# A three-stage attention and mixture kernel: weight mixing moved into the attention loop, query loads put ahead of value loads, keys stored once per tile

## The chip, the cores and the metric

The kernel runs on one core of a Trainium2 chip. The metric is the device time of one execution in microseconds (us); lower is better.

## What is computed

The reference is three stages, each feeding the next. Cut to what matters:

```python
# 1. chunked attention, B=2, H=8, S=768, D=64, with 8 memory keys
for c in range(S // 32):
    q_c = q[:, :, c*32:(c+1)*32]
    k_ctx = k[:, :, max(0, c*32-16):min(S, c*32+32+8)]     # v_ctx likewise
    k_full = np.concatenate([mem_k, k_ctx], axis=2)        # 64 keys
    scores = scale * np.matmul(q_c, k_full.transpose(0, 1, 3, 2))
    scores = scores - np.max(scores, axis=-1, keepdims=True)
    a = np.exp(scores); a = a / (np.sum(a, axis=-1, keepdims=True) + 1e-09)
    out[:, :, c*32:(c+1)*32] = np.matmul(a, v_full)
# 2. channel mixing, x is (2, 768, 512)
xk = mu_k * x + (1.0 - mu_k) * x_prev                      # xr likewise
k = np.maximum(xk @ w_k, 0.0)                              # 512 -> 1024
out = sigmoid(xr @ w_r) * (k * k @ w_v)                    # 512 -> 512, 1024 -> 512
# 3. top-1 of 8 experts per token, with a sequential rule for keeping the last expert
h = np.maximum(x[b, s] @ w1[e], 0.0); out[b, s] = p[e] * (h @ w2[e])
```

## The kernel before

The 1536 tokens are 12 tiles of 128 rows. Each engine has its own instruction stream, written out by hand, and the streams meet at semaphores; there is no scheduler. Pairs of tiles are one round of a loop: `over_pairs` runs round 0, then rounds 1 to 4 as a loop, then round 5. `u` (0 or 1) is the tile's place in its pair and picks the buffer.

**Attention, one tile t.** TensorE (PE) transposes the probabilities of tile t (`probs_transposed`, L343, four 128x128 transposes), computes the scores of tile t+2 (`scores`, L330), transposes the normalised output of tile t-1 (`x_transposed`, L368) and multiplies probabilities by values (`values`, L357). Scores and values are 32 small matmuls each, of 64 rows and 32 columns of the array; a fp32 matmul leaves two records in the trace. VectorE (DVE) takes maxima and subtracts them (`shifted`, L765 and L775), then normalises (`normed`, L784, L790, L795). ScalarE (ACT) copies the transposed probabilities out of PSUM (L576), copies the transposed output (L582) and takes the exponentials of tile t+2 (L570).

**Its loads.** SyncE (SP) issues all of them in order on one queue. `QK` holds a tile's queries (512 words a partition) and keys. The keys are laid out by the host as four windows of 64 keys for each head pair, 8 memory keys and 56 others in each, so neighbouring windows repeat keys: 1024 words. `VV` holds the values, 1040 words. Both have two buffers. `QK` of tile t+4 may be loaded when the scores of tile t+2 are done, and `VV` of tile t+2 when `values` of tile t is done; SP waits for the second first:

```python
def ahead(t, u, more=True):
    sp.wait_ge(pv_done, t + 1)
    v_load(t + 2, u)
    if more:
        sp.wait_ge(scores_done, t + 3)
        qk_load(t + 4, u)
```

`probs_transposed` of tile t waits for the exponentials of t, `VV` of t and, in all but the last pair, `QK` of t+2.

**Weights of the channel mixing.** They come as 10 chunks of 128x1024 (`RAW`, two buffers, from `wmix`). ACT rounds each into `WHI` (`weight_hi`, L588) and DVE subtracts to get `WLO` (`weight_lo`, L805); each product is then three matmuls, high by high, high by low and low by high. The ten loads are queued behind the last value load. Four chunks are converted in the last attention pair, two after each tile; the other six inside the first round of the mixing. The products there are `up` (L403), `gate` (L419), `down` (L435). The mixing's inputs are made by ACT (`mix_scaled`, L616; `mix_hi`, L627) and DVE (`mix_full`, L812; `mix_lo`, L820). For pair 0 this stands in the last attention pair, behind the first tile's two weight chunks, and ahead of the copy L576 that the last tile's `values` needs. `up` waits for four chunks of `WLO` and for the last copy L582. Later `x2_transposed` (L445) needs `X2F` from DVE (L876), and `logits` (L453) are four fp32 matmuls with a 128x128 stationary operand and nine moving columns.

**Constants.** `CO` (940 words a partition) holds the identity used by all transposes and the tables of the routing. Every engine waits for all of it, and for two small tensors that ACT loads, `MU` and `WG` (`const_in` at 48).

**Experts.** After the routing, each expert's weights are loaded, split and multiplied (L513, L530). The change leaves this stage alone.

Of the kernel before, what the change touches and what calls it, by code (L numbers as in the profile page):

```python
# [33 lines left out]
VW = DH + 1  # L34
QW, KW, VWT = HP * P, HP * CPT * KEYS, HP * CPT * VW
INW = QW + KW + VWT
NPAIR = NT // 2
# [22 lines left out]
def moe_program(nc, tiles, wmix, mus, wgate, wexp, consts, out):  # L60
    ctx = ExitStack()
    with ctx:
# [58 lines left out]

        QK = [place(f"QK{i}", [P, QW + KW]) for i in range(2)]
        VV = [place(f"VV{i}", [P, VWT]) for i in range(2)]
# [32 lines left out]

        const_in = sem("const_in")
        qk_loaded = [sem(f"qk_loaded{i}") for i in range(2)]
        v_loaded = [sem(f"v_loaded{i}") for i in range(2)]
# [83 lines left out]
        @block.sync  # L243
        def _(sp):
            def qk_load(t, u):
                sp.dma_start(QK[u][:], tiles[ds(t, 1), :, 0:QW + KW].rearrange("a p n -> (a p) n")
                             ).then_inc(qk_loaded[u], 16)

            def v_load(t, u):
                sp.dma_start(VV[u][:], tiles[ds(t, 1), :, QW + KW:INW].rearrange("a p n -> (a p) n")  # L250
                             ).then_inc(v_loaded[u], 16)

            def raw_load(n, u):
                sp.dma_start(RAW[u][:], wmix[:, ds(n * CH1, CH1)]).then_inc(raw_loaded[u], 16)

            qk_load(0, 0)
            sp.dma_start(CO[:], consts).then_inc(const_in, 16)
            qk_load(1, 1)
            v_load(0, 0)
            v_load(1, 1)  # L260

            def ahead(t, u, more=True):

                sp.wait_ge(pv_done, t + 1)
                v_load(t + 2, u)
                if more:
                    sp.wait_ge(scores_done, t + 3)
                    qk_load(t + 4, u)

            for t in range(2):  # L270
                sp.wait_ge(scores_done, t + 1)
                qk_load(t + 2, t)
            with sp.Fori(0, NPAIR - 2) as g:
                ahead(2 * g, 0)
                ahead(2 * g + 1, 1)
# [38 lines left out]
        def _(pe):  # L314
# [3 lines left out]
            def scores(t, u, first):  # L318
# [5 lines left out]
                q = QK[u][:, 0:QW].rearrange("p (h n) -> p h n", h=HP)  # L324
                k = QK[u][:, QW:QW + KW].rearrange("p (h c n) -> p h c n", h=HP, c=CPT)
# [61 lines left out]

            pe.wait_ge(wlo_done, N1A)
            pe.wait_ge(xt_evac, NT)
# [18 lines left out]
            def gate(g, u, first):  # L408
                pe.wait_ge(xlo_done[1], g + 1)
                if first:  # L410
                    pe.wait_ge(wlo_done, N1A + KT * D // CH1)
                else:
                    pe.wait_ge(sig_done, 2 * g + u - 1)
# [10 lines left out]
            def down(g, u, first):  # L424
# [4 lines left out]
                for f in range(FT):  # L429
                    c = WV0 + f * D  # L430
                    if first and c % CH1 == 0:
                        pe.wait_ge(wlo_done, c // CH1 + 1)
                    r = slice(u * P, u * P + P)
# [46 lines left out]


            pe.wait_ge(route_step, R_FLAGS)
            nc.tensor.transpose(PS[0][0:NT, 0:P], RN[3][:], ident)
# [81 lines left out]
        def _(act):  # L565
# [19 lines left out]

            def weight_hi(n):
                act.wait_ge(raw_loaded[n % 2], 16 * (n // 2 + 1))
                nc.scalar.activation(WHI[:, n * CH1:(n + 1) * CH1], RAW[n % 2][:],  # L588
                                     ACT.Copy).then_inc(whi_done, 1)

            def attention(g, first, last):
                for u in range(2):
# [69 lines left out]
            def mix(g, first, last):  # L662
# [97 lines left out]
        def _(dve):  # L760
# [40 lines left out]

            def weight_lo(n):
                dve.wait_ge(whi_done, n + 1)
                c = slice(n * CH1, (n + 1) * CH1)
                nc.vector.tensor_tensor(WLO[:, c], RAW[n % 2][:], WHI[:, c].bitcast(F32),  # L805
                                        ALU.subtract).then_inc(wlo_done, 1)
# [16 lines left out]
            def attention(g, first, last):  # L823
                for u in range(2):
# [14 lines left out]
            nc.vector.tensor_scalar(OM[:], MU[:], -1.0, 1.0, ALU.mult, ALU.add)  # L839
            nc.vector.tensor_copy(X2R[:, :, D + 1], CO[:, C_TOK:C_TOK + NT])  # L840
            nc.vector.memset(ZR[:, 0:D + 1], 0.0)
# [36 lines left out]
            def mix(g, first, last):  # L878
                squared(g, 0, first)
                if not first:  # L880
                    logits_out(2 * g - 2)
                if first:
                    weight_lo(N1A)
                squared(g, 1, first)
                if not first:
                    logits_out(2 * g - 1)
                else:
                    weight_lo(N1A + 1)
                squared(g, 2, first)
                if first:  # L890
                    weight_lo(N1A + 2)
                squared(g, 3, first)
                if first:
                    for n in range(N1A + 3, N1):
                        weight_lo(n)
                if not last:
# [241 lines left out]
def _layout(q, k, v, mem_k, mem_v):  # L1138
# [5 lines left out]
    qt = q.reshape(B, HP, 2, ntb, P, DH).transpose(0, 3, 2, 5, 1, 4).reshape(NT, P, QW)  # L1144
    kw = np.empty((B, H, nch, KEYS, DH), k.dtype)
    vw = np.zeros((B, H, nch, KEYS, VW), v.dtype)
    kw[:, :, :, :] = mem_k[:, :, None, 0:1]
    for c in range(nch):
        lo, hi = max(0, c * CHUNK - LEFT), min(S, (c + 1) * CHUNK + RIGHT)
        at = NMEM + lo - (c * CHUNK - LEFT)  # L1150
        kw[:, :, c, 0:NMEM] = mem_k
        kw[:, :, c, at:at + hi - lo] = k[:, :, lo:hi]
# [4 lines left out]
    kt = kw.reshape(B, HP, 2, ntb, CPT, KEYS, DH).transpose(0, 3, 2, 6, 1, 4, 5).reshape(NT, P, KW)  # L1157
    vt = vw.reshape(B, HP, 2, ntb, CPT, KEYS, VW).transpose(0, 3, 2, 5, 1, 4, 6).reshape(NT, P, VWT)
    return np.ascontiguousarray(np.concatenate([qt, kt, vt], axis=2))

# [49 lines left out]
```

## Time and profile before

| what | value |
|---|---|
| median of 3 runs | 531.41 us (528.64 to 531.82) |
| profiled execution | 533.26 us, its span 531.5 us |
| busy in the span | PE 440.0, DVE 245.9, ACT 212.7, POOL 55.3 us |
| mean granted TensorE clock | 0.919 of 2.4 GHz |
| moved by DMA | 67.31 MB |

The span runs from the first to the last instruction of the profiled execution; its own time is 1.8 us longer. Times within the trace count from the span's start. A granted clock of 1.00 is 2.4 GHz and 0.50 is 1.2 GHz. The chain of waits follows the last instruction back to what released it; an entry there is work or a transfer that nothing hid. A DMA's entry in it starts at its issue and ends when it has landed.

### The profile page before, as it was taken

Reading aid. Unit: us, or ns where it says so; the run is one execution under the profiler, and the core shown is the slowest. Engines: PE = TensorE matmul, PEld = TensorE weight load, DVE = VectorE, ACT = ScalarE, POOL = GpSimd, SP = SyncE. Lnnn points to the kernel's source line nnn. Section 1 sums busy time; section 2 is a strip of 40 time slices with the busy share of each in tenths; the row PEclk is TensorE's granted clock in tenths of the full one; section 3 lists DMA queues with packets and bytes.
Section 4 is the critical chain, followed back from the end, with each engine's and each line's share of the span. In section 5 each row is a group of like instructions: output and inputs, shape, how many; then the busy total and the mean of one; then the engine's idle time right before and its main releaser. Section 6 shows DMA issues by size and latency. Waiting matters only on the chain.

```text
span 531.5 us, 10141 instructions
## 1 busy us (share of the span) xinstructions
PE 440.0 (83%) x3759; PEld 366.4 (69%) x3759; DVE 245.9 (46%) x477; ACT 212.7 (40%) x319; POOL 55.3 (10%) x62
## 2 busy tenths in 40 slices
PE   1667628999999999999940069999999999999993
PEld 1545518889898989989830047777777777777772
DVE  2454575653535234354045149222382247464861
ACT  1333474663435253344022038222462245555750
POOL 0000000010100101010003601111111111111110
PEclk9967867999999999999975569999999999999998
DMA  8668442428000000000004779511173128383810
GB/s 302 253 208 294 157 181 86 152 90 309 0 0 0 0 0 0 0 0 1 2 0 158 238 281 406 209 54 40 52 227 136 40 71 253 141 251 132 271 61 10
DMA packets 18313, 67.31 MB, mean 127 GB/s; under 512 B 2734, under 2 KB 2734, under 8 KB 18288
## 3 DMA queue, kind: packets, MB, share of 16 engines
q1 hardware_dynamic: 13104, 50.92, 27.9%
q0 software_dynamic: 4896, 16.05, 8.8%
q8 instruction: 15, 0.25, 0.2%
q14 instruction: 10, 0.08, 0.0%
q10 hardware_dynamic: 288, 0.02, 0.0%
HBM read 55.41 MB, written 12.62 MB: 128 GB/s over the span
## 4 chain that ended last, share of the span: by engine, by line
PE 67%; DMA 14%; issue 7%; DVE 5%; POOL 3%; ACT 2%; SPq 1%; POOLq 0%; DVEq 0%; ACTq 0%
PE PS L530 16%; PE PS L403 12%; PE PS L513 12%; PE PS L435 10%; DMA QK<-tiles 5%; PE PS L419 5%; DMA XR<-grouped_rows 5%; POOL grouped_rows L1107 2%; PE PS L521 2%; PE PS L453 2%; PE PS L504 1%; PE PS L330 1%; PE PS L357 1%; DMA RAW<-wmix 1%; PE PS L343 1%
## 5 line engine op out<-in xcount | busy, mean ns | idle before, releaser
L1022 DVE TENSOR_TENSOR ELO<-ERAW,EHI 128x1024 fp32r<-128x1024 f32 x56 | 66.8, 1219 | 12.9 <-ACT EHI L696 10.3
L696 ACT ACTIVATE EHI<-ERAW 128x1024 fp32r<-128x1024 f32 x56 | 57.4, 1053 | 29.6 <-DMA ERAW<-wexp 20.8
L403 PE MATMUL PS<-XHI,WHI 128*128 128x256 f32 x192 | 56.6, 295 | 1.2 <-DVE WLO L805 1.2
L530 PE MATMUL PS<-EHI,HH 128*128 128x512 f32 x128 | 54.6, 426 | 2.6 <-issue 1.0
L403 PE MATMUL PS<-XHI,WLO 128*128 128x256 f32 x192 | 55.2, 287 | 0.0
L403 PE MATMUL PS<-XLO,WHI 128*128 128x256 f32 x192 | 55.1, 287 | 0.0
L513 PE MATMUL PS<-EHI,XSH 128*128 128x512 f32 x128 | 53.0, 414 | 1.4 <-DVE XSL L1030 1.4
L1043 DVE TENSOR_TENSOR HL<-PS,HH 128x512 fp32r<-128x512 f32 x32 | 22.1, 691 | 66.3 <-ACT HH L716 65.9
L513 PE MATMUL PS<-ELO,XSH 128*128 128x512 f32 x128 | 51.5, 402 | 0.0
L513 PE MATMUL PS<-EHI,XSL 128*128 128x512 f32 x128 | 51.2, 400 | 0.0
L530 PE MATMUL PS<-EHI,HL 128*128 128x512 f32 x128 | 50.6, 395 | 0.0
L530 PE MATMUL PS<-ELO,HH 128*128 128x512 f32 x128 | 50.5, 395 | 0.0
L857 DVE TENSOR_TENSOR KK<-KR 128x512 f32<-128x512 f32 x24 | 16.6, 692 | 53.3 <-ACT KR L643 53.2
L1123 POOL DMA_INDIRECT rows_out<-OSB,OIDX x16 | 20.4, 1274 | 185.0 <-DVE OIDX L1077 185.0
L711 ACT ACTIVATE HS<-PS 128x512 f32<-128x512 f32 x32 | 19.1, 596 | 50.0 <-PE PS L513 50.0
L403 PEld LDWEIGHTS PS<-XHI,WHI 128*128 128x128 f32 x192 | 37.7, 196 | 1.6 <-issue 1.6
L403 PEld LDWEIGHTS PS<-XHI,WLO 128*128 128x128 f32 x192 | 37.8, 197 | 0.0
L403 PEld LDWEIGHTS PS<-XLO,WHI 128*128 128x128 f32 x192 | 37.7, 196 | 0.0
L435 PE MATMUL PS<-WHI,KHI 128*128 128x512 f32 x96 | 37.5, 390 | 0.1
L435 PE MATMUL PS<-WHI,KLO 128*128 128x512 f32 x96 | 37.4, 389 | 0.0
L435 PE MATMUL PS<-WLO,KHI 128*128 128x512 f32 x96 | 37.3, 389 | 0.0
L504 PE MATMUL PS<-CO,XR 128*128 128x128 f32 x68 | 10.9, 284 | 31.1 <-DMA XR<-grouped_rows 31.1
(141 smaller groups left out, 774.6 us busy)
## 6 DMA issues: line engine op xcount, KB each, us to landing
ERAW<-wexp SPq DMA_DIRECT2D x56, 512.0 KB, 5.6
QK<-tiles SPq DMA_DIRECT2D x12, 768.0 KB, 5.7
VV<-tiles SPq DMA_DIRECT2D x12, 520.0 KB, 3.9
grouped_rows<-ZR POOLq DMA_DIRECT2D x1, 5140.0 KB, 18.1
RAW<-wmix SPq DMA_DIRECT2D x10, 512.0 KB, 3.8
XR<-grouped_rows POOLq DMA_DIRECT2D x17, 257.0 KB, 4.2
CO<-consts SPq DMA_DIRECT2D x1, 470.0 KB, 6.5
rows_out<-OSB,OIDX POOLq DMA_INDIRECT x16, 3.9
```

The source lines that it names most:

```text
L403: last = nc.tensor.matmul(PS[q % 2][:, half * 256:half * 256 + 256], w[:, c:c + P], x[:, k, :], start=n == 0, stop=n == 11)
L419: last = nc.tensor.matmul(PS[2 + u][:, :], x[:, k, r], w[:, c:c + D], start=n == 0, stop=n == 11)
L435: last = nc.tensor.matmul(PS[4 + u][:, :], x[:, f, r], w[:, c:c + D], start=n == 0, stop=n == 23)
L504: last = nc.tensor.transpose(PS[5][:, k * P:(k + 1) * P], XR[:, k * P:(k + 1) * P], ident)
L513: last = nc.tensor.matmul(PS[part][:, :], x[:, k, :], ww[:, c:c + 512], start=n == 0, stop=n == 11)
L530: last = nc.tensor.matmul(PS[4][:, :], x[:, f, :], ww[:, c:c + D], start=n == 0, stop=n == 23)
L696: nc.scalar.activation(EHI[w][:, c * CH2:(c + 1) * CH2], ERAW[c][:], ACT.Copy).then_inc(ehi_done, 1)
L711: nc.scalar.activation(HS[:, part * 512:part * 512 + 512], PS[part][:, :], ACT.Relu).then_inc(hrelu_done, 1)
L857: nc.vector.tensor_tensor(KK[q % 2][:], KR[q % 2][:], KR[q % 2][:], ALU.mult).then_inc(kk_done, 1)
L1022: nc.vector.tensor_tensor(ELO[w][:, c * CH2:(c + 1) * CH2], ERAW[c][:], EHI[w][:, c * CH2:(c + 1) * CH2].bitcast(F32), ALU.subtract).then_ ...
L1043: nc.vector.tensor_tensor(HL[:, 4 * part:4 * part + 4, :].rearrange("p k n -> p (k n)"), PS[2 + part][:, :], HH[:, 4 * part:4 * part + 4, ...
L1123: pool.indirect_dma_start(out, bass.IndirectOffsetOnAxis(ap=OIDX[:, 0:1], axis=0), OSB[:], None, bounds_check=last_row, oob_is_err=False). ...
```

## The change

All 10 chunks are converted in the attention: one `weight_hi` and one `weight_lo` at the end of each tile from tile 2 on, with one `RAW` load per tile behind that tile's value load. In SP's loop the query load now stands first. A tile's keys are stored once (152 per head, `KWIN`) and its 8 memory keys once per head; each 32-row chunk reads its 56 keys as a window of the 152. The memory keys are multiplied by eight matmuls of their own, one per head, with all 128 queries of the tile as stationary operand and 8 moving columns, ahead of the 32 small ones, which now have 56 columns. `QK` has 1152 words a partition, not 1536. Only the identity (128 words) of `CO` is loaded at the start; the tables follow behind the last `RAW` load under a semaphore of their own.

```diff
-QW, KW, VWT = HP * P, HP * CPT * KEYS, HP * CPT * VW
-INW = QW + KW + VWT
+KWIN = LEFT + P + RIGHT
+QW, KW, MW, VWT = HP * P, HP * KWIN, HP * NMEM, HP * CPT * VW
+QKW = QW + KW + MW
+INW = QKW + VWT
...
             qk_load(0, 0)
-            sp.dma_start(CO[:], consts).then_inc(const_in, 16)
+            sp.dma_start(CO[:, 0:C_LT], consts[:, 0:C_LT]).then_inc(const_in, 16)
...
-            def ahead(t, u, more=True):
-
+            def raw_next(n, u):
+
+                sp.wait_ge(wlo_done, n + 1)
+                raw_load(n, u)
+
+            def ahead(t, u):
+
+                sp.wait_ge(scores_done, t + 3)
+                qk_load(t + 4, u)
                 sp.wait_ge(pv_done, t + 1)
                 v_load(t + 2, u)
-                if more:
-                    sp.wait_ge(scores_done, t + 3)
-                    qk_load(t + 4, u)
+                raw_next(t, u)
...
-            ahead(NT - 4, 0, False)
-            ahead(NT - 3, 1, False)
-            for n in range(N1):
-                if n >= 2:
-                    sp.wait_ge(wlo_done, n - 1)
-                raw_load(n, n % 2)
+            for u in range(2):
+                sp.wait_ge(pv_done, NT - 3 + u)
+                v_load(NT - 2 + u, u)
+                raw_next(N1 - 2 + u, u)
+            sp.dma_start(CO[:, C_LT:CW], consts[:, C_LT:CW]).then_inc(tables_in, 16)
...
+                for hp in range(HP):
+                    for par in range(2):
+                        r = slice(DH * par, DH * par + DH)
+                        nc.tensor.matmul(PS[2 * u + par][:, hp * KEYS:hp * KEYS + NMEM], q[r, hp, :], m[r, hp, :],
+                                         start=True, stop=True)
...
-                                PS[2 * u + par][CHUNK * c:CHUNK * (c + 1), hp * KEYS:(hp + 1) * KEYS],
-                                q[r, hp, c * CHUNK:(c + 1) * CHUNK], k[r, hp, c, :], start=True, stop=True)
+                                PS[2 * u + par][CHUNK * c:CHUNK * (c + 1), hp * KEYS + NMEM:(hp + 1) * KEYS],
+                                q[r, hp, c * CHUNK:(c + 1) * CHUNK],
+                                k[r, hp, c * CHUNK:c * CHUNK + KEYS - NMEM], start=True, stop=True)
...
-            pe.wait_ge(wlo_done, N1A)
+            pe.wait_ge(wlo_done, N1A + 2)
...
-                    if last:
-                        for n in (2 * u, 2 * u + 1):
-                            weight_hi(n)
+                    if not first:
+                        weight_hi(t - 2, u)
...
-                    if first:
-                        weight_hi(N1A + q - 1)
                     relu_square(g, q, first)
-                if first:
-                    for n in range(N1A + 3, N1):
-                        weight_hi(n)
...
-                    if last:
-                        for n in (2 * u, 2 * u + 1):
-                            weight_lo(n)
+                    if not first:
+                        weight_lo(t - 2, u)
...
+            dve.sem_inc(wlo_done, 2)
```

The six `weight_lo` of the first mixing round go as well, and DVE copies the token numbers from the tables there (one 128x12 copy) where it did so at the very start before. The host layout of the keys changes to match.

SP in the attention loop, one tile. Before:

```order
L250 ISA [waits pv_done]
L250 DMA VV_93<-tiles 128x1040
L267 REGISTER_ALU
L246 ISA [waits scores_done]
L246 DMA QK_91<-tiles 128x1536
```

and now:

```order
L249 ISA [waits scores_done]
L249 DMA QK_91<-tiles 128x1152
L274 REGISTER_ALU
L253 ISA [waits pv_done]
L253 DMA VV_93<-tiles 128x1040
L257 ISA [waits wlo_done]
L257 DMA RAW_89<-wmix 128x1024
```

The query load has moved ahead of the wait for `values`, and a third load with a wait on DVE's `weight_lo` stands behind the value load.

PE in the attention loop, from the probabilities' transposes to the output's. Before:

```order
L343 MATMUL PS<-CO,PR_97 128x128 x3
L330 MATMUL PS<-QK_91 32x64 [waits sub_done,const_in]
L330 MATMUL PS<-QK_91 32x64 x31
L366 REGISTER_ALU [waits norm_done]
L368 MATMUL PS<-CO,XN_102 128x128 [waits xt_evac]
```

and now:

```order
L357 MATMUL PS<-CO,PR_97 128x128 x3
L337 MATMUL PS<-QK_91 128x8 [waits sub_done,const_in]
L337 MATMUL PS<-QK_91 128x8 x7
L343 MATMUL PS<-QK_91 32x56 x32
L380 REGISTER_ALU [waits norm_done]
L382 MATMUL PS<-CO,XN_102 128x128 [waits xt_evac]
```

Eight matmuls of 128x8 have come in between the transposes and the scores; the 32 behind them are eight columns narrower.

ACT in the last attention pair, from the first tile's copies to the second tile's. Before:

```order
L576 ACTIVATE PTS_99<-PS 128x512 [waits pv_done,pt_done]
L582 ACTIVATE XT<-PS 128x4x128 [waits xt_done,const_in]
L588 ACTIVATE WHI<-RAW_89 128x1024 [waits raw_loaded0]
L588 ACTIVATE WHI<-RAW_90 128x1024 [waits raw_loaded1]
L616 ACTIVATE XF_83<-XT,MU 128x256 [waits xt_evac,const_in]
L616 ACTIVATE XF_83<-XT,MU 128x256 x3
L616 ACTIVATE XF_84<-XT,MU 128x256 [waits xt_evac,const_in]
L616 ACTIVATE XF_84<-XT,MU 128x256 x3
L627 ACTIVATE XHI_85<-XF_83 128x1024 [waits xfk_done]
L627 ACTIVATE XHI_86<-XF_84 128x1024 [waits xfr_done]
L576 ACTIVATE PTS_100<-PS 128x512 [waits pv_done,pt_done]
```

and now:

```order
L591 ACTIVATE PTS_99<-PS 128x512 [waits pv_done,pt_done]
L597 ACTIVATE XT<-PS 128x4x128 [waits xt_done,const_in]
L604 ACTIVATE WHI<-RAW_89 128x1024 [waits raw_loaded0,const_in]
L631 ACTIVATE XF_83<-XT,MU 128x256 [waits xt_evac,const_in]
L631 ACTIVATE XF_83<-XT,MU 128x256 x3
L631 ACTIVATE XF_84<-XT,MU 128x256 [waits xt_evac,const_in]
L631 ACTIVATE XF_84<-XT,MU 128x256 x3
L642 ACTIVATE XHI_85<-XF_83 128x1024 [waits xfk_done]
L642 ACTIVATE XHI_86<-XF_84 128x1024 [waits xfr_done]
L591 ACTIVATE PTS_100<-PS 128x512 [waits pv_done,pt_done]
```

One of the two conversions is gone from this place.

## Rows read from the trace of the kernel before

**Rows 1.** Stages: width, busy (count) PE, PEld, DVE, ACT, POOL; clock, DMA share, GB/s

```profile
0.00:14.80 14.80, 2.35 (x128) 1.95 (x129) 3.74 (x15) 2.43 (x3) 0.20 (x4) 1.00 0.84 304
14.80:64.25 49.45, 35.47 (x1357) 27.63 (x1357) 25.31 (x85) 16.46 (x29) 0.00 (x0) 0.79 0.65 230
64.25:82.91 18.66, 5.45 (x148) 4.06 (x149) 13.90 (x29) 12.60 (x21) 0.00 (x0) 0.66 0.44 145
82.91:113.42 30.51, 30.36 (x168) 26.80 (x168) 17.20 (x24) 18.75 (x27) 0.00 (x0) 0.93 0.33 103
113.42:270.00 156.58, 154.54 (x978) 139.67 (x977) 59.58 (x105) 58.90 (x103) 12.08 (x13) 1.00 0.09 34
```

**Rows 2.** Waits in total in the attention loop, 14.8 to 64.25: us, times, longest

```profile
PE PS L343 <- DMA QK<-tiles: 17.8, 8, 4.3
```

**Rows 3.** Chain of waits: start, us, what (start-up, then one pair of tiles)

```profile
9.08 5.59 DMA QK<-tiles
...
44.37 5.24 DMA QK<-tiles
...
49.86 1.09 PE PS L343 x4
...
53.10 0.89 PE PS L357 x53
...
54.68 5.18 DMA QK<-tiles
```

**Rows 4.** Timeline of PE, one tile at full clock: start, us, what

```profile
44.16 0.63 PE L343 MATMUL PS<-CO,PR 128*128 128x128 f32 x4 [0.48 <-DMA QK<-tiles]
...
46.10 0.86 PE L357 MATMUL PS<-VV,PTS 64*32 64x65 f32 x64
```

**Rows 5.** DMA issues: count, KB each, median us from issue to landing

```profile
QK<-tiles SPq DMA_DIRECT2D x12, 768.0 KB, 5.7
VV<-tiles SPq DMA_DIRECT2D x12, 520.0 KB, 3.9
...
CO<-consts SPq DMA_DIRECT2D x1, 470.0 KB, 6.5
...
WG<-wgate ACTq DMA_DIRECT2D x1, 18.0 KB, 5.5
```

**Rows 6.** A stretch with the queue never empty, columns as in rows 1

```profile
46.00:49.00 3.00, 0.96 (x66) 0.70 (x64) 2.22 (x9) 1.23 (x2) 0.00 (x0) 1.00 1.03 402
```

**Rows 7.** Chain of waits: the logits of one tile in the channel mixing

```profile
117.61 0.80 PE PS L453 x8
```

**Rows 8.** Groups by line, count, busy, mean ns, idle before: conversions, then attention

```profile
L805 DVE TENSOR_TENSOR WLO<-RAW,WHI 128x1024 fp32r<-128x1024 f32 x10 | 12.1, 1223 | 6.5 <-ACT WHI L588 6.5
...
L588 ACT ACTIVATE WHI<-RAW 128x1024 fp32r<-128x1024 f32 x10 | 10.4, 1055 | 6.4 <-DMA RAW<-wmix 6.2
...
L765 DVE TENSOR_REDUCE MX<-PS 128x4 f32<-128x256 f32 x16 | 6.0, 419 | 14.3 <-PE PS L330 14.2
L775 DVE TENSOR_TENSOR SX<-PS,MX 128x256 f32<-128x256 f32 x16 | 6.0, 419 | 0.9
...
L570 ACT ACTIVATE PR<-SX 128x512 f32<-128x512 f32 x8 | 5.0, 624 | 0.9 <-DVE SX L775 0.9
```

**Rows 9.** Timeline from the last attention pair to the first `up`, [idle before <-releaser]

```profile
69.12 1.06 ACT L588 ACTIVATE WHI<-RAW 128x1024 fp32r<-128x1024 f32 x1 [2.21 <-DMA RAW<-wmix]
...
73.08 3.27 DVE L812 SCALAR_TENSOR_TENSOR XF<-XT,OM,XF 128x256 f32<-128x256 f32 x8 [0.37 <-ACT XF L616]
...
76.38 1.06 ACT L627 ACTIVATE XHI<-XF 128x1024 fp32r<-128x1024 f32 x1 [0.54 <-DVE XF L812]
...
78.02 1.19 PE L357 MATMUL PS<-VV,PTS 64*32 64x65 f32 x64 [9.00 <-issue]
...
81.77 0.60 ACT L582 ACTIVATE XT<-PS 128x512 f32<-128x512 f32 x1 [1.47 <-PE PS L368]
...
82.91 0.55 PE L403 MATMUL PS<-XHI,WHI 128*128 128x256 f32 x1 [1.24 <-DVE WLO L805]
```

**Rows 10.** Waits of PE in the channel mixing, 82 to 270

```profile
PE PS L445 <- DVE X2F L876: 0.7, 1, 0.7
```

More of the change, by code:

```diff
@@ L120, in moe_program @@
         inner = top[0]
-        QK = [place(f"QK{i}", [P, QW + KW]) for i in range(2)]
+        QK = [place(f"QK{i}", [P, QKW]) for i in range(2)]
         VV = [place(f"VV{i}", [P, VWT]) for i in range(2)]
@@ L157, in moe_program @@
         const_in = sem("const_in")
+        tables_in = sem("tables_in")
         qk_loaded = [sem(f"qk_loaded{i}") for i in range(2)]
@@ L245, in qk_load @@
             def qk_load(t, u):
-                sp.dma_start(QK[u][:], tiles[ds(t, 1), :, 0:QW + KW].rearrange("a p n -> (a p) n")
+                sp.dma_start(QK[u][:], tiles[ds(t, 1), :, 0:QKW].rearrange("a p n -> (a p) n")
                              ).then_inc(qk_loaded[u], 16)
             def v_load(t, u):
-                sp.dma_start(VV[u][:], tiles[ds(t, 1), :, QW + KW:INW].rearrange("a p n -> (a p) n")
+                sp.dma_start(VV[u][:], tiles[ds(t, 1), :, QKW:INW].rearrange("a p n -> (a p) n")
                              ).then_inc(v_loaded[u], 16)
@@ L324, in scores @@
                 q = QK[u][:, 0:QW].rearrange("p (h n) -> p h n", h=HP)
-                k = QK[u][:, QW:QW + KW].rearrange("p (h c n) -> p h c n", h=HP, c=CPT)
+                k = QK[u][:, QW:QW + KW].rearrange("p (h n) -> p h n", h=HP)
+                m = QK[u][:, QW + KW:QKW].rearrange("p (h n) -> p h n", h=HP)
+                for hp in range(HP):
[3 more added lines that the diff above has]
+                                         start=True, stop=True)
                 for hp in range(HP):
@@ L410, in gate @@
                 if first:
-                    pe.wait_ge(wlo_done, N1A + KT * D // CH1)
+                    pe.wait_ge(wlo_done, N1A + KT * D // CH1 + 2)
                 else:
@@ L431, in down @@
                     if first and c % CH1 == 0:
-                        pe.wait_ge(wlo_done, c // CH1 + 1)
+                        pe.wait_ge(wlo_done, c // CH1 + 3)
                     r = slice(u * P, u * P + P)
@@ L479, in _ @@
             logits(NT - 1, 1)
+            pe.wait_ge(tables_in, 16)
             pe.wait_ge(route_step, R_FLAGS)
@@ L584, in x_out, with weight_hi @@
                                      ACT.Copy).then_inc(xt_evac, 1)
-            def weight_hi(n):
-                act.wait_ge(raw_loaded[n % 2], 16 * (n // 2 + 1))
-                nc.scalar.activation(WHI[:, n * CH1:(n + 1) * CH1], RAW[n % 2][:],
+            def weight_hi(n, u):
+                act.wait_ge(const_in, 48)
+                act.wait_ge(raw_loaded[u], 8 * (n - u) + 16)
+                nc.scalar.activation(WHI[:, ds(n * CH1, CH1)], RAW[u][:],
                                      ACT.Copy).then_inc(whi_done, 1)
@@ L800, in normed, with weight_lo @@
                 last.then_inc(norm_done, 1)
-            def weight_lo(n):
+            def weight_lo(n, u):
+                dve.wait_ge(const_in, 48)
                 dve.wait_ge(whi_done, n + 1)
-                c = slice(n * CH1, (n + 1) * CH1)
-                nc.vector.tensor_tensor(WLO[:, c], RAW[n % 2][:], WHI[:, c].bitcast(F32),
+                nc.vector.tensor_tensor(WLO[:, ds(n * CH1, CH1)], RAW[u][:], WHI[:, ds(n * CH1, CH1)].bitcast(F32),
                                         ALU.subtract).then_inc(wlo_done, 1)
@@ L839, in _ @@
             nc.vector.tensor_scalar(OM[:], MU[:], -1.0, 1.0, ALU.mult, ALU.add)
-            nc.vector.tensor_copy(X2R[:, :, D + 1], CO[:, C_TOK:C_TOK + NT])
             nc.vector.memset(ZR[:, 0:D + 1], 0.0)
@@ L881, in mix @@
                     logits_out(2 * g - 2)
-                if first:
-                    weight_lo(N1A)
                 squared(g, 1, first)
@@ L886, in mix @@
                     logits_out(2 * g - 1)
-                else:
-                    weight_lo(N1A + 1)
                 squared(g, 2, first)
                 if first:
-                    weight_lo(N1A + 2)
+                    dve.wait_ge(tables_in, 16)
+                    nc.vector.tensor_copy(X2R[:, :, D + 1], CO[:, C_TOK:C_TOK + NT])
                 squared(g, 3, first)
-                if first:
-                    for n in range(N1A + 3, N1):
-                        weight_lo(n)
                 if not last:
@@ L1144, in _layout @@
     qt = q.reshape(B, HP, 2, ntb, P, DH).transpose(0, 3, 2, 5, 1, 4).reshape(NT, P, QW)
-    kw = np.empty((B, H, nch, KEYS, DH), k.dtype)
+    kw = np.empty((B, H, ntb, KWIN, DH), k.dtype)
+    kw[:] = mem_k[:, :, None, 0:1]
+    for i in range(ntb):
+        lo, hi = max(0, i * P - LEFT), min(S, (i + 1) * P + RIGHT)
+        kw[:, :, i, lo - (i * P - LEFT):hi - (i * P - LEFT)] = k[:, :, lo:hi]
     vw = np.zeros((B, H, nch, KEYS, VW), v.dtype)
-    kw[:, :, :, :] = mem_k[:, :, None, 0:1]
     for c in range(nch):
@@ L1150, in _layout @@
         at = NMEM + lo - (c * CHUNK - LEFT)
-        kw[:, :, c, 0:NMEM] = mem_k
-        kw[:, :, c, at:at + hi - lo] = k[:, :, lo:hi]
         vw[:, :, c, 0:NMEM, 0:DH] = mem_v
@@ L1156, in _layout @@
         vw[:, :, c, at:at + hi - lo, DH] = 1.0
-    kt = kw.reshape(B, HP, 2, ntb, CPT, KEYS, DH).transpose(0, 3, 2, 6, 1, 4, 5).reshape(NT, P, KW)
+    kt = kw.reshape(B, HP, 2, ntb, KWIN, DH).transpose(0, 3, 2, 5, 1, 4).reshape(NT, P, KW)
+    mt = mem_k.reshape(B, 1, HP, 2, NMEM, DH).repeat(ntb, 1).transpose(0, 1, 3, 5, 2, 4).reshape(NT, P, MW)
     vt = vw.reshape(B, HP, 2, ntb, CPT, KEYS, VW).transpose(0, 3, 2, 5, 1, 4, 6).reshape(NT, P, VWT)
-    return np.ascontiguousarray(np.concatenate([qt, kt, vt], axis=2))
+    return np.ascontiguousarray(np.concatenate([qt, kt, mt, vt], axis=2))
 def _blocks(w):
```

## The prediction

> **What bounds the kernel now.** I first read the busy shares by stage [rows 1]. From 113.42 us on PE is busy 154.5 of 156.6 us at full clock, and in the first mixing round, 82.91 to 113.42, 30.36 of 30.51. Nothing that frees ACT or DVE there can shorten it by more than its small holes. The two stretches before are different: in the attention, 14.80 (first transposes of tile 0) to 64.25 (first transposes of tile 10), PE is busy 35.5 of 49.45, DVE 25.3, ACT 16.5, DMA 0.65; in the passage to the mixing, 64.25 to 82.91, PE works 5.5 of 18.7 us. So the change can act on some 83 us of the 531.5, and the question is what waits there.
>
> In the attention, PE waited for a `QK` load 8 times, 17.8 us in total [rows 2]. The chain of waits shows the loop it closes [rows 3]: the load issued at 44.37 takes 5.24, the transposes start at 49.86, `values` ends at 53.99, the next load is issued at 54.68 and takes 5.18. Two tiles take 10.3 us; over the ten tiles of the stretch it is 4.95 a tile. `values` is in this loop although the `QK` buffer does not need it: SP waits for it first, and only then issues the query load. The transfer itself is not the limit. With the queue never empty the DMAs move 402 GB/s [rows 6], so the 1.32 MB of a tile need 3.3 us of its 4.95.
>
> In the passage, three things queue: ACT waits 2.21 for the first `RAW`, converts two chunks, makes the inputs of pair 0, and only after the second `mix_hi` (76.38) copies the probabilities that `values` has waited 9.00 us for; later `up` waits 1.24 for `WLO` [rows 9].
>
> **The change part by part.** The sum is made against the profiled execution, 533.26 us; the median of the runs shown is 1.85 lower, and I move the difference onto it.
>
> *Start.* Before the first scores PE waits for `QK` 0 and `CO`, 786 + 481 KB, which landed at 7.8 us. Now it is 590 + 66 KB, 0.61 MB less, 1.5 us at 402 GB/s. `WG` is awaited too and lands 5.5 after its issue at 1.3 [rows 5], so at 6.8: only 1.0 is gained. Then come eight memory-key matmuls that were not there (below, 0.8 to 1.6), so the scores of tile 0 end about when they did, and `QK` 2 is issued at about 9.1 again. It then took 5.59 [rows 3] with some 0.7 MB still ahead of it (3.12 MB asked for, moved at 0.40 MB/us from about 3 us on) and 0.79 of its own; now 2.31 MB are asked for before it, gone by 8.8. I take 4.1: the 3.9 of a 520 KB load [rows 5] plus 0.15 for its 590 KB. Tile 0 begins 1.6 earlier; 2.4 if the constants land with `QK`, 0.6 if the load still queues. **-1.6**.
>
> *Memory keys.* Per tile 8 matmuls, 16 records. The nearest row is the logits, also fp32 with a 128-column stationary operand and few moving columns: 8 records in 0.80 us at full clock [rows 7], 0.10 each. So 1.6 a tile if they run one after the other. They alternate between the two halves of the rows, as the scores do; halved, 0.8. The 32 scores matmuls lose 8 of 64 columns; from nothing to 0.1. PE's tile takes 2.80 at full clock (44.16 to 46.96) [rows 4] and becomes 3.6 to 4.4. I take 4.0. The Trainium skill, "TensorE: Matmul & The Clock Gate", Part 3, says that weight loads overlap running matmuls only where the row group differs, which would make it 0.8, PE's tile 3.6 and the forecast about 1 us lower; no row here shows such a pair with 128 columns.
>
> *Query load first, smaller.* Now SP issues `QK` t+4 about 0.4 after the scores of t+2. A 590 KB load takes 4.1 alone and 5.4 behind one `RAW` (524 KB, 1.3). Round the loop, two tiles: 0.4 + 5.4 + 0.25 + transposes and scores (half of 2.80, plus 1.2) 2.6 = 8.65, against 10.3. SP also stands at the wait for `WLO` before the next query load; I add 0.5: 9.15, 4.6 a tile.
>
> *What is late next.* Four loops come close together. (a) The value load: `values` of t, then `VV` of t+2, issue 0.4, landing 3.9 [rows 5] to 5.2 behind a `RAW`, 0.25, and PE's whole tile of 4.0: 8.6 to 9.9 for two tiles, 4.3 to 4.9. (b) Bytes: 590 + 532 + 524 KB a tile is 1.65 MB, 4.1 us at 402 GB/s [rows 6]. (c) ACT and DVE in turn: exponentials 0.62, `WHI` 1.06, `WLO` 1.22, the two maxima and two subtractions of the next tile 4 x 0.42 = 1.68 [rows 8]: 4.6 round, since ACT converts behind the exponentials, DVE subtracts behind the conversion, and the next `shifted` stands behind that on DVE. (d) PE 4.0. The cover of the moved conversions is thus nearly used up: ACT goes from 1.65 to 2.7 a tile, DVE from 2.5 to 3.75, and no engine is full, but the order ties them. With four loops between 4.0 and 4.6 and some jitter I take **4.7** a tile, 47.0 for the ten: **-2.45**. Bounds 4.4 (the loops overlap well) and 5.1 (each value load behind a `RAW`): -5.45 and +1.55.
> The rows show the DMAs at 402 to 420 GB/s when the queue is full. The Trainium skill, "DMA: Bandwidth & Descriptors", Specifications, gives about 358 GB/s as the memory's limit for a core. By that figure, an estimate, loop (b) would be 4.6 and the loads, not the order, would bound the attention; the row goes against the figure, and the measurement decides.
>
> *Passage.* The wait for `RAW` and one conversion are gone from ACT ahead of `mix_scaled` (2.21 + 0.2 + 1.06 = 3.5), but the copy for tile 10 now stands behind a conversion (about 1 later), its `values` and `normed` follow, and DVE's `WLO` 8 and `mix_full` behind these; `mix_hi` waited for `mix_full` already (0.54) [rows 9]. So 2.5 to 3.3 are left at the second `mix_hi`: 2.9. At its end `WLO` 9 is one subtraction, not two, and is over before the last copy (81.77 + 0.60 = 82.37), which `up` now waits for instead of 82.91: 0.5. **-3.4**, from -2.9 to -4.0. The half-clock start of `up` stays, since PE is still idle ahead of it.
>
> *First mixing round.* Six conversions and subtractions leave ACT and DVE, and PE was hardly waiting: 0.15 within, and 0.7 for `X2F` [rows 10], which DVE made late because the conversions had held up the next inputs. **-0.9**, from -0.7 to -1.2. The remaining waits (`wlo_done`) are met at once, and the tables are asked for in the last attention pair, far ahead of their first reader. The copy of token numbers, 0.17, is hidden there as it was at the start. Nothing reaches the experts.
>
> Sum: -1.6 - 2.45 - 3.4 - 0.9 = -8.35. From 533.26 that is 524.9, and on the median 523.1. With all bounds at their low ends 518.4, with all at their high ends 528.8.
>
> **The rivals.** (1) *Slower.* The memory-key matmuls cost PE more than the loads gave back. The attention ran at a mean clock of 0.79 [rows 1]: transposes take 0.63 at full [rows 4] and 1.09 at half [rows 3], and the tile from 49.86 to 53.99, largely at half, took 4.13. If PE stays at half and the eight matmuls run one after the other, 1.6 to 3.2 come on top: about 6.2 a tile, 62 for the ten, +12.5. With -0.6, -3.4 and -0.9 elsewhere it gives 539. It decides from 5.5 a tile on. For it: PE was at half clock while busy three quarters of the time. Against: at 6.2 a tile it would be busy without a gap, and `up` ran at half for only some 4 us before it rose.
> (2) *The wait is only exchanged.* The query load goes out earlier but lands behind a `RAW` and a value load, and SP, held at the wait for `WLO`, issues the next ones late: 5.2 a tile, +2.5, with -5.9 elsewhere: 528.0. For it: six loads on one queue and 25% more bytes a tile. Against: the queue was empty a third of the time.
> (3) *All loops overlap* and the memory keys cost 0.8 or less: 4.3 a tile, -6.45, with -5.9: 519.1.
>
> **How the numbers follow.** Forecast 0.53, (1) 0.12, (2) 0.20, (3) 0.15. The predicted time is the forecast's, 523.1. The range is 516.5 to 531.0: it takes in (2) and (3) with some 3 us beside each for the start and the passage, and leaves out (1). About 1% (5.3 us) is what a measurement of this kernel can tell from no change. Below 526.1 lie the most of the forecast (0.48), (3), and a little of (2): 0.68. Within 1% the rest of both: 0.20. Slower 0.12.
>
> **What the changed profile would show.** The step on the loads is right if the two-tile distance of the transposes is 9 to 9.8 us instead of 10.3 and PE's waits for `QK` fall well below 17.8; right on the order if the query load's issue follows the scores by less than 0.6. The memory keys' records should take 0.8 to 1.6 a tile. ACT should reach `mix_scaled` without a wait for `RAW`, `up` should start about 7.5 earlier than 82.91, and the wait of 0.7 for `X2F` be gone. From there to the end the lengths should be the same. The prediction is wrong if the tile takes 5.5 or more, if the clock in the loop stays at half, or if the mixing or the experts become longer or shorter.

## The result: slower by 0.9%, outside the forecast range

The changed kernel took 536.0 us in the median (533.0 to 539.3), the kernel before 531.4; the ratio is 1.0087 with a 95% interval from 1.0053 to 1.0122. The forecast was 523.1 in a range from 516.5 to 531.0. A second set of ten executions gave 536.1 (1.0087, 1.0053 to 1.0120). One execution of halves_in_turn below took 546.6 us, over 1.5% above the fastest of its kernel, and is left out of its median.

The profiled execution took 533.02 us, the fastest of the first set, while that of the kernel before, 533.26, lay 1.85 above its median. So the two traces show the causes better than the sum. The stages of the changed kernel, columns as in [rows 1]; the edges are the same events (first transposes of tiles 0 and 10, first `up`, first transposes of `X2F`):

```profile
0.00:12.86 12.86, 5.75 (x160) 5.41 (x161) 3.76 (x14) 1.93 (x3) 0.20 (x4) 1.00 0.72 238
12.86:70.78 57.92, 50.57 (x1516) 42.16 (x1517) 33.93 (x94) 23.05 (x37) 0.00 (x0) 0.76 0.75 248
70.78:85.80 15.02, 6.93 (x148) 5.03 (x149) 12.42 (x27) 11.39 (x19) 0.00 (x0) 0.55 0.36 128
85.80:115.27 29.47, 29.47 (x168) 26.60 (x169) 11.77 (x20) 12.72 (x21) 2.09 (x2) 0.94 0.04 13
```

Start 1.9 us shorter, passage 3.6, first mixing round 1.7: 7.3 in all, and the ten tiles of the attention 8.5 longer, 57.92 against 49.45. PE was busy 35.5 us of the loop before and is now 50.6. In the second trace of the same kernel the loop took 58.84 and the mixing's first round ended at 117.09 instead of 115.27 (before: 114.08): 3.0 and 1.2 us later than before. What follows that point is all but the same code in every kernel here and took 416.0 to 420.5 us in their traces, so single traces don't add up to the 4.6 of the medians.

What PE waits for in the loop now (us in total, times, longest):

```profile
PE PS L357 <- DMA VV<-tiles: 2.0, 2, 1.8
PE PS L357 <- ACT PR L585: 1.8, 3, 1.0
PE PS L357 <- DMA QK<-tiles: 1.6, 1, 1.6
...
PE PS L337 <- issue: 1.3, 1, 1.3
PE PS L371 <- issue: 1.0, 1, 1.0
```

The wait for the query load is gone, 1.6 instead of the 17.8 of [rows 2], and nothing of its size has come in its place: PE itself is the bound. The chain of waits says with what. Start, us, what:

```profile
38.01 1.09 PE PS L357 x4
39.10 1.81 PE PS L337 x16
40.91 1.03 PE PS L343 x64
41.94 1.04 PE PS L382 x4
42.99 1.12 PE PS L371 x63
44.11 0.99 PE PS L357 x4
45.10 0.99 PE PS L337 x16
```

L337 is the eight memory-key matmuls. At 39.10, at half clock (1.2 GHz), they are the longest step of a tile that is 6.1 us of PE work from end to end; at 45.10, at full clock (2.4 GHz), they take 0.99. The chain runs on PE alone through such a tile, where before it ran through a load [rows 3]. And the clock did not rise with the work. One stretch, columns as in the stages:

```profile
28.00:45.00 17.00, 15.57 (x377) 12.54 (x376) 9.88 (x28) 7.01 (x11) 0.00 (x0) 0.50 0.74 233
```

PE was busy 15.57 of 17 us and stayed at 1.2 GHz. By the clock and the durations together, PE ran at half clock for about 39 of the loop's 58 us (12.9 to 24.4, 27.8 to 44.9, 51.7 to 62.0), and before for about 25 of 49. In the second trace the same stretch shows 0.60 with PE busy 14.19. The starts of the transposes (L357), from the timeline, give the tile at either clock:

```profile
31.51 1.11 PE L357 MATMUL PS<-CO,PR 128*128 128x128 f32 x4
...
38.01 1.09 PE L357 MATMUL PS<-CO,PR 128*128 128x128 f32 x4 [0.38 <-ACT PR L585]
...
44.05 1.05 PE L357 MATMUL PS<-CO,PR 128*128 128x128 f32 x4
...
49.28 0.63 PE L357 MATMUL PS<-CO,PR 128*128 128x128 f32 x4 [1.05 <-ACT PR L585]
...
62.03 0.63 PE L357 MATMUL PS<-CO,PR 128*128 128x128 f32 x4 [0.36 <-ACT PR L585]
...
66.00 0.63 PE L357 MATMUL PS<-CO,PR 128*128 128x128 f32 x4 [0.20 <-DMA VV<-tiles]
...
70.78 0.63 PE L357 MATMUL PS<-CO,PR 128*128 128x128 f32 x4 [1.02 <-DMA VV<-tiles]
```

Two tiles at half clock took 6.50 and 6.04 us. Three that ran almost wholly at full clock took 5.23, 3.97 and 4.78, 4.66 in the mean. Three are few, and the last two stand where fewer query loads are left.

The loads land as follows (KB each, median us from issue to landing), and then what SP waited for in the first 75 us (us in total, times, longest):

```profile
QK<-tiles SPq DMA_DIRECT2D x12, 576.0 KB, 4.7
VV<-tiles SPq DMA_DIRECT2D x12, 520.0 KB, 5.3
...
RAW<-wmix SPq DMA_DIRECT2D x10, 512.0 KB, 4.6
```

```profile
SPq L249 <- PE PS L343: 21.3, 8, 5.1
SPq L257 <- DVE WLO L815: 20.3, 8, 3.7
SPq L253 <- PE PS L371: 12.1, 10, 3.0
```

The value load has gone from 3.9 [rows 5] to 5.3, behind a query load and with a `RAW` load around it. SP still finds time to wait for the scores (L249, 21.3), so its stand at `WLO` hardly held the queries back.

### The profile page after: what moved, and what is told of

It is laid out like the page before. It is cut to its first block, busy times and chain, and to the rows that moved or that the text cites. A ratio compares the mean times of both kernels' runs of the same rounds, so it can differ in the third digit from the quotient of the medians.

```text
span 531.3 us, 10579 instructions
## 1 busy us (share of the span) xinstructions
PE 458.5 (86%) x3951; PEld 384.3 (72%) x3951; DVE 246.2 (46%) x477; ACT 211.5 (40%) x319; POOL 54.3 (10%) x62
## 4 chain that ended last, share of the span: by engine, by line
PE 77%; DMA 7%; issue 6%; DVE 4%; POOL 3%; ACT 1%; SPq 0%; ACTq 0%; DVEq 0%; POOLq 0%
PE PS L545 16%; PE PS L417 13%; PE PS L528 13%; PE PS L449 12%; PE PS L433 6%; DMA XR<-grouped_rows 3%; PE PS L337 3%; POOL grouped_rows L1110 2%; PE PS L536 2%; PE PS L467 2%; PE PS L357 2%; PE PS L382 2%; PE PS L343 2%; PE PS L519 1%; DMA VV<-tiles 1%
## 5 line engine op out<-in xcount | busy, mean ns | idle before, releaser
L545 PE MATMUL PS<-EHI,HL 128*128 128x512 f32 x128 | 50.6, 395 | 0.0
L519 PE MATMUL PS<-CO,XR 128*128 128x128 f32 x68 | 10.9, 285 | 29.7 <-DMA XR<-grouped_rows 29.7
```

The costliest lines, as they stand in the source:

```text
L519: last = nc.tensor.transpose(PS[5][:, k * P:(k + 1) * P], XR[:, k * P:(k + 1) * P], ident)
L545: last = nc.tensor.matmul(PS[4][:, :], x[:, f, :], ww[:, c:c + D], start=n == 0, stop=n == 23)
```

## The experiments

Twelve runs. Per tile is the distance of the first transposes of tiles 0 and 10 divided by ten; passage and first mixing round as in the stages above; us of one trace each. The last two columns are medians and the ratio to the kernel before, measured again beside each set of runs (530.9 to 531.9 us); the ratio comes from all these executions and isn't exactly that of two medians.

| kernel | tile 0 at | per tile | passage | first mixing | median us | ratio (95%) |
|---|---|---|---|---|---|---|
| before | 14.80 | 4.95 | 18.66 | 31.17 | 531.4 | 1 |
| changed | 12.86 | 5.79 | 15.02 | 29.47 | 536.0 | 1.0087 (1.0053 to 1.0122) |
| changed_again | 12.83 | 5.88 | 14.98 | 30.44 | 536.1 | 1.0087 (1.0053 to 1.0120) |
| windows_kept | 14.41 | 5.17 | 14.73 | 30.64 | 528.2 | 0.9939 (0.9909 to 0.9969) |
| keys_only | 14.54 | 5.78 | 18.95 | 31.45 | 539.8 | 1.0173 (1.0120 to 1.0226) |
| memory_twice | 14.54 | 6.78 | 15.17 | 29.81 | 547.0 | 1.0336 (1.0266 to 1.0406) |
| order_only | 14.95 | 4.62 | 18.27 | 31.80 | 528.4 | 0.9947 (0.9920 to 0.9973) |
| weights_only | 15.12 | 5.40 | 15.56 | 29.47 | 531.4 | 1.0003 (0.9977 to 1.0030) |
| waits_at_use | 13.59 | 4.70 | 15.71 | 29.71 | 525.7 | 0.9902 (0.9874 to 0.9930) |
| loads_only | 14.37 | 4.08 | 17.46 | 31.22 | 522.4 | 0.9846 (0.9816 to 0.9876) |
| filled | 12.97 | 5.87 | 17.06 | 30.13 | 537.1 | 1.0105 (1.0066 to 1.0144) |
| no_memory | 12.03 | 4.89 | 14.78 | 30.40 | 525.9 | 0.9889 (0.9840 to 0.9939) |
| chunks_early | 13.95 | 4.19 | 14.74 | 30.86 | 520.5 | 0.9789 (0.9745 to 0.9833) |
| halves_in_turn | 13.69 | 6.04 | 14.82 | 30.04 | 538.4 | 1.0156 (1.0071 to 1.0241) |

**First four: which part costs.** Theory 1 is that the memory-key matmuls bind PE, theory 2 that the third load on SP's queue does.

*windows_kept* takes the key change back:

```diff
-KWIN = LEFT + P + RIGHT
-QW, KW, MW, VWT = HP * P, HP * KWIN, HP * NMEM, HP * CPT * VW
-QKW = QW + KW + MW
+QW, KW, VWT = HP * P, HP * CPT * KEYS, HP * CPT * VW
+QKW = QW + KW
...
-                        nc.tensor.matmul(PS[2 * u + par][:, hp * KEYS:hp * KEYS + NMEM], q[r, hp, :], m[r, hp, :],
-                                         start=True, stop=True)
```

> The changed kernel with the keys as before: four windows of 64 keys a head pair, no memory-key matmuls, 768 KB query loads. Theory 1, the memory-key matmuls bind PE in the attention: without them PE needs 2.8 us a tile at full and about 4.2 at half clock, the bytes (1.84 MB a tile at 402 GB/s) 4.6, so 4.7 to 5.0 a tile against 5.8, and 523 to 527 us in all. Theory 2, the third load on SP's queue and its wait bind the attention: with still more bytes a tile it stays at 5.8 or more, 536 to 540 us.

528.2: 7.9 us under the changed kernel although it loads 0.2 MB more a tile. Theory 1 holds; but 5.17 a tile and 528.2 are both a little above what it expected, and the waits say that theory 2 names what is next:

```profile
PE PS L349 <- DMA VV<-tiles: 12.6, 7, 3.0
PE PS L349 <- DMA QK<-tiles: 5.2, 1, 5.2
```

*keys_only* is the reverse, the kernel before with the new `QK`, the new host layout and the new `scores` body, and nothing else.

> The kernel before with the new key layout and the eight memory-key matmuls a tile alone. Theory 1: PE gets 1.0 us (full clock) to 1.8 us (half) more a tile in the loop that runs through the query load, which itself is about 0.5 shorter a pair: 5.5 to 6.4 a tile, 537 to 544 us. Theory 2: the smaller loads help or do nothing, 527 to 531 us.

539.8, ratio 1.0173: the key change alone costs 8.1 us, 0.83 a tile, as much as taking it back gave. No third load is in this kernel, and PE was busy 51.7 of the loop's 57.8 us.

*memory_twice*:

```diff
-                for hp in range(HP):
+                for hp in [h for h in range(HP) for _ in range(2)]:
                     for par in range(2):
                         r = slice(DH * par, DH * par + DH)
                         nc.tensor.matmul(PS[2 * u + par][:, hp * KEYS:hp * KEYS + NMEM], q[r, hp, :], m[r, hp, :],
```

> The changed kernel with each memory-key matmul issued twice (the second writes the same values). Theory 1: 1.0 to 1.8 us more a tile in 12 tiles, 12 to 22 us over the changed kernel, 548 to 558 us. Theory 2: PE has room while the loads are late, at most 3 us more, 536 to 539 us.

547.0: 11 us more, 0.99 a tile, just under theory 1's range and far over theory 2's 3. Had PE had room, the second set would have been free.

*order_only*:

```diff
+                if more:
+                    sp.wait_ge(scores_done, t + 3)
+                    qk_load(t + 4, u)
                 sp.wait_ge(pv_done, t + 1)
                 v_load(t + 2, u)
-                if more:
-                    sp.wait_ge(scores_done, t + 3)
-                    qk_load(t + 4, u)
```

> The kernel before with the query load ahead of the value load in SP's loop, nothing else. Both theories let the query load go out some 2 us earlier; the value load is next: 4.6 to 4.9 a tile instead of 4.95, 528 to 531 us. If the query load's place was what cost, it is 527 or less; if the value load takes over at once, 531 or more.

528.4, 3.3 us faster, 4.62 a tile. The new order of the loads is a gain. That 4.62 is also the prediction's figure for this loop is in part chance: it was worked out for a smaller query load behind a `RAW` load, and here the load is 768 KB and there is no `RAW`.

**Next four: the weights, the value load, the clock.** *weights_only* is windows_kept with the value load ahead of the query load again and all of `CO` at the start:

```diff
-                sp.wait_ge(scores_done, t + 3)
-                qk_load(t + 4, u)
                 sp.wait_ge(pv_done, t + 1)
                 v_load(t + 2, u)
+                sp.wait_ge(scores_done, t + 3)
+                qk_load(t + 4, u)
                 raw_next(t, u)
```

> The kernel before with the weight mixing in the attention loops alone: keys, constants and the order value load before query load as before, the RAW load behind both. The conversions find room on ACT and DVE, so what they cost is the third load: 5.2 to 5.5 us a tile instead of 4.95, +2.5 to +5.5, against 3.5 less in the passage and 1 to 1.5 less in the first mixing round: 529 to 533 us. If the conversions themselves blocked DVE or ACT, the tile would be 5.8 and more, 535 or above.

531.4, no difference (1.0003). The gains came, 3.1 in the passage and 1.7 in the first mixing, and the loop took 4.5 of them back: PE waits for the query load 21.2 us instead of 17.8 (us in total, times, longest):

```profile
PE PS L347 <- DMA QK<-tiles: 21.2, 8, 4.6
```

*waits_at_use* moves PE's wait for a tile's values from the probabilities' transposes to the output's, two steps later:

```diff
             def probs_transposed(t, u, first, more):
                 pe.wait_ge(exp_done, t + 1)
-                pe.wait_ge(v_loaded[u], 8 * (t - u) + 16)
...
             def x_transposed(t, u, first):
+                if not isinstance(t, int) or t < NT - 1:
+                    pe.wait_ge(v_loaded[1 - u], 8 * (t + u) + 16)
```

> windows_kept with one wait moved: PE waits for a tile's value load ahead of the transposes of the output, behind the scores, and no longer ahead of the transposes of the probabilities. If the value load behind the RAW load is what bound windows_kept (12.6 us of waits, 7 times), a tile falls from 5.17 to 4.6 to 4.9 us and the time to 522 to 526 us. If the bytes bind it (1.84 MB a tile), it stays at 527 to 529.

525.7 and 4.70 a tile against windows_kept's 5.17: the value load was the bound there, because PE waited for it two steps before it needed it. The bytes were not: 1.84 MB a tile need 4.6 us at the 402 GB/s of [rows 6]. At 4.70 they are close, though, with the DMAs busy 0.89 of the loop.

*loads_only* keeps the conversions and keys of before and rearranges loads: order_only, the moved wait, only the identity of `CO` at the start, and in SP's tail

```diff
+            for u in range(2):
+                sp.wait_ge(pv_done, NT - 3 + u)
+                v_load(NT - 2 + u, u)
+                raw_load(u, u)
+            sp.dma_start(CO[:, C_LT:CW], consts[:, C_LT:CW]).then_inc(tables_in, 16)
+            for n in range(2, N1):
```

> The kernel before with its loads reordered alone: query load first, the wait for values moved as in waits_at_use, the first two RAW loads ahead of the end of the attention, the tables of CO loaded after them. Keys and the place of the conversions as before. Against order_only (528.4): 2.2 less in the passage, 1 to 2 less at the start, up to 2 in the loop: 523 to 526 us. If the passage was not bound by the wait for RAW, 526 to 528.

522.4, below its range, with 4.08 a tile: more than the moved wait was expected to give. Two parts of the expectation missed: against order_only the passage is 0.8 shorter and not 2.2 (17.46 against 18.27), and tile 0 begins 0.6 earlier and not 1 to 2.

*filled* puts wide matmuls, that no result uses, among PE's small ones:

```diff
                     pe.wait_ge(xt_evac, t)
+                for _ in range(8):
+                    nc.tensor.matmul(PS[7][:, 0:256], CO[:, 0:64].bitcast(mybir.dt.bfloat16),
+                                     CO[:, 0:128].bitcast(mybir.dt.bfloat16), start=True, stop=True)
```

> The changed kernel with eight bf16 matmuls of 128x128 by 128x256 a tile ahead of the output's transposes, into a PSUM bank that these overwrite. They are 0.11 us each at full clock and 0.21 at half. If the half clock is what makes the memory keys dear and wide matmuls raise it: PE's tile is 3.9 + 0.9 = 4.8 us instead of 6.1, 5.0 to 5.3 a tile, 528 to 532 us. If the clock stays where it was: 1.7 more a tile, 550 to 556 us.

The clock rose and the time didn't fall: 537.1 lies between the two expected ranges. The same stretch as above, and one row of the timeline:

```profile
28.00:45.00 17.00, 15.66 (x486) 13.27 (x484) 10.52 (x30) 7.69 (x12) 0.00 (x0) 0.87 0.68 223
```

```profile
27.07 1.88 PE L337 MATMUL PS<-QK 64*128 64x8 f32 x16 [2.18 <-issue]
```

PE is as busy as in the changed kernel, 15.66 against 15.57 us, at 0.87 instead of 0.50. The fillers are the only difference in the program, so in these two traces the busy share alone doesn't account for the clock. What the higher clock gave went to the eight fillers (0.9 a tile), to a 2.18 us stall in the loop's first round and to longer waits for the value load (5.2 us in the loop instead of 2.0); how much of the 10 us the half clock is worth by itself this run doesn't say.

**Last four.** *no_memory* leaves the memory keys out of the result; the 32 matmuls have 64 columns and read eight other words in their place.

```diff
-                        nc.tensor.matmul(PS[2 * u + par][:, hp * KEYS:hp * KEYS + NMEM], q[r, hp, :], m[r, hp, :],
-                                         start=True, stop=True)
...
+                            k0 = QW + hp * KWIN + c * CHUNK
...
+                                QK[u][r, k0:k0 + KEYS], start=True, stop=True)
```

> The changed kernel without its eight memory-key matmuls a tile: the 32 scores matmuls take 64 columns again and read the eight words behind their 56 keys in place of the memory keys, so the memory keys are left out of the result. Loads as in the changed kernel (576 KB). Theory 1, the eight matmuls cost and the smaller load helps: 4.6 to 5.0 a tile, 523 to 526 us, below windows_kept (528). If the smaller load brings nothing because the value load binds: 527 to 529. If it is something else in the key change: 533 or more.

525.9. With the changed kernel this splits the key change: the eight matmuls cost 10.1 us, and against windows_kept the smaller loads gave 2.3. The second figure is not clear of the noise: the intervals of the two ratios overlap.

*changed_again* is the changed kernel unchanged.

> The changed kernel once more, for a second trace and more times. Expected 534 to 538 us, first transposes of tile 10 at 70 to 73 us of the span; if the attention is what the 4.6 us come from, the length from the first transposes of the first mixing round's output on is within 1.5 us of that before.

536.1; tile 10 at 71.67, and from the first transposes of `X2F` to the end 417.91 against 417.42 before. The attention is where the loss lies: its loop is 8.5 and 9.4 us longer in the two traces.

*chunks_early* is loads_only with the first two weight chunks in tiles 0 and 1 and the next two in tiles 10 and 11:

```diff
+            raw_load(0, 0)
+            raw_load(1, 1)
...
-                    if last:
-                        for n in (2 * u, 2 * u + 1):
-                            weight_hi(n)
+                    if first or last:
+                        weight_hi(u if first else 2 + u)
```

> loads_only with weight chunks 0 and 1 loaded behind the fourth query load and converted in tiles 0 and 1, where the DMAs were idle and DVE waits, and chunks 2 and 3 one after each of the last two tiles. Against loads_only (522.4): one conversion and subtraction less in the passage, 1 to 2.5 us, and 0 to 1 more in tiles 1 to 3: 520 to 522 us. If the added loads delay the query load of tile 4, 523 to 524.

520.5, ratio 0.9789 (0.9745 to 0.9833): faster than both kernels, 11 us below the one before, with a passage of 14.74 as in the changed kernel and 4.19 a tile.

*halves_in_turn* swaps the two loops around the memory-key matmul, so that four use the upper rows of the array and then four the lower.

> The changed kernel with its eight memory-key matmuls in another order: four on the upper half of the rows, then four on the lower, instead of alternating. If the alternation lets the weight loads of one half overlap the other's matmuls, the 16 records go from 0.99 us at full clock towards 1.6 (0.10 each, as the logits), from 1.8 to 2.0 or more at half, 2 to 7 us more in all: 538 to 543 us. If it does not matter, 0.99 and 1.8 stay and the time is the changed kernel's, 535 to 537.

538.4, which alone is hardly apart from the changed kernel (533.0 to 539.3). The records decide. The 16 take, at half and at full clock:

```profile
42.42 2.75 PE L337 MATMUL PS<-QK 64*128 64x8 f32 x16
49.35 1.53 PE L337 MATMUL PS<-QK 64*128 64x8 f32 x16
```

against 1.88 and 1.06 in the changed kernel. Alternating the halves hides a third of the price. PE was busy 28.17 of the 29 us from 20 to 49 here, and the durations are those of half clock up to 49: a second case of a busy PE at 1.2 GHz. The Trainium skill, "TensorE: Matmul & The Clock Gate", Part 3, says that weight loads overlap running matmuls only where the row group differs; the runs agree in kind, with a third saved and not the half that the prediction's lower end supposed.

## Why the prediction was wrong, step by step

**What bounds the kernel: right.** The stages that moved lay ahead of 115 us and were the ones it named.

**Start, -1.6: came as -1.9,** by another way. The constants landed at 5.4, not 6.8, and the memory-key matmuls took 1.88, more than the 0.8 to 1.6 allowed:

```profile
5.47 1.88 PE L337 MATMUL PS<-QK 64*128 64x8 f32 x16 [5.47 <-DMA CO<-consts]
```

`QK` 2 was then issued at 8.41, not 9.1, and took 4.31, not 4.1. That the errors nearly cancel is luck.

The stage row reads a granted clock of 1.00 there, and so did [rows 1] for 0 to 14.8. The durations are those of half clock: the transposes at 12.86 take 1.09, as at 14.80 before. Ahead of the first rise near 24 us (19 before) the clock row is not to be believed.

**Memory keys, "PE's tile ... becomes 3.6 to 4.4. I take 4.0": this step failed.** The price from the logits was right at full clock, 0.99 for 16 records, between its two ends. It was taken at full clock alone. At half it is 1.81, the other four steps 4.3, and PE's tile 6.1. Over the ten tiles PE was busy 5.06 a tile, not 4.0, and the loop took 5.8, not 4.7: +8.5 in this trace where -2.45 was forecast, 10.9 us apart; forecast and result differ by 12.9. The three tiles at full clock, 4.66 in the mean, would have borne the 4.7 out, so it is the clock that the sum had wrong. The reason for passing over the half clock stood in rival (1): "at 6.2 a tile it would be busy without a gap", so the clock would rise. The stretch from 28 to 45 us refutes it. In filled, with eight wide matmuls a tile more, the same stretch has the same busy share and a clock of 0.87. The Trainium skill, "TensorE: Matmul & The Clock Gate", section "Loop structure matters more than you think", says that the loop nest decides whether matmuls stay warm, back-to-back ones keeping the clock up; this loop ran nearly back to back (15.57 of 17.00 us) at half clock, so the trace doesn't bear it out for small matmuls. Rival (1) is what happened, at 5.8 instead of 6.2 a tile; it had a chance of 0.12 and ended outside the range. Its point of decision, 5.5 a tile, was right.

**Query load first: right in kind.** PE's wait for `QK` fell from 17.8 to 1.6 us in the changed kernel, in part because PE itself was slower there. Order_only, the new order alone, took 4.62 a tile; the forecast of 4.6 was for other loads, as said above.

**What is late next: right in kind, unused.** Loop (a), the value load behind a `RAW`, bound windows_kept (12.6 us) and its bound of 5.1 was nearer than 4.7: rival (2), which priced this exchange of waits at 5.2 a tile, fits windows_kept's 5.17, without the memory keys. Loop (b) was no bound: waits_at_use moved 1.84 MB a tile in 4.70, and the changed kernel moves 1.65 in 5.79. Loop (c) showed no wait of weight: ACT and DVE were busy 23.1 and 33.9 of 57.9 us, and DVE waited 1.4 for `WHI`. SP's wait for `WLO` (20.3 us) seems to have replaced waiting that it would have done for the scores; no run took it away alone.

**Passage, -3.4: -3.6.** Timeline, with idle before and releaser:

```profile
73.41 1.05 ACT L604 ACTIVATE WHI<-RAW 128x1024 fp32r<-128x1024 f32 x1
...
76.44 3.25 DVE L822 SCALAR_TENSOR_TENSOR XF<-XT,OM,XF 128x256 f32<-128x256 f32 x8
...
79.72 1.06 ACT L642 ACTIVATE XHI<-XF 128x1024 fp32r<-128x1024 f32 x1 [0.53 <-DVE XF L822]
...
81.36 1.18 PE L371 MATMUL PS<-VV,PTS 64*32 64x65 f32 x64 [4.76 <-issue]
...
85.80 0.55 PE L417 MATMUL PS<-XHI,WHI 128*128 128x256 f32 x1 [0.80 <-issue]
```

`WHI` has no wait for `RAW` now (2.21 in [rows 9]), and `up` no wait for `WLO`.

**First mixing round, -0.9: -1.7** in this trace, -0.7 in the second. The wait for `X2F` is gone from both.

**The conversions.** Forecast as a gain of 4.3 in passage and mixing, with the loop still 2.45 shorter than before. weights_only shows 4.8 gained and 4.5 given back in the loop, where PE's waits for the query load grew. This is the second term that was mis-sized, hidden behind the first.

## What to carry to other kernels

A matmul with few moving columns isn't cheap for that: in the changed loop the eight with 8 columns and a 128-column stationary operand kept PE busy for 14.9 us, the 32 with 56 columns and a 32-column one for 9.7. That the width of the stationary operand, which has to be loaded, sets the price would fit; no run varied it. The eight bought a query load smaller by 25%, and cost 10.1 us where the smaller load gave some 2. Price new work on TensorE at both clocks, and don't count on the clock rising because the engine is busy: here it stayed at 1.2 GHz through 17 us of small matmuls. Before bytes are saved, look at which wait stands earlier than its use and in which order the loads are asked for: moving one wait and a few loads gave 8.6 us here without touching the arithmetic.

## What the runs showed that was not expected

PE at 92% busy (15.57 of 17.00 us) stayed at 1.2 GHz with fp32 matmuls of 8, 56, 65 and 128 columns, and was at a mean of 0.87 with eight bf16 ones of 256 columns a tile among them. It is one trace of each.

Early in the attention loop PE stood still for nothing that the profile shows: 1.30 and 1.04 us in the changed kernel, 1.93 in order_only, 2.18 in filled, 2.81 and 1.59 in waits_at_use, 1.99 in loads_only. Before and in weights_only there was none, but PE waited for query loads there. One of the DMA queues in the profile carries instructions (5 packets, 0.08 MB in the changed loop), and the DMAs were at 0.88 in the changed kernel's longer stall, so that the fetching of the loop's code waited behind the loads would fit. But keys_only stood still for 1.53 us, from 29.88 to 31.41, while the DMAs moved nothing (share 0.00, 0 GB/s). So loads in the way are not the whole cause, and it stays open.
